# Softmax of the tap weights in three parts, two of them among the first products

## The reference, cut to what matters

```python
# x: (2, 3584, 192); weight_gen: (2, 3584, 8, 7)
w = weight_gen - np.max(weight_gen, axis=-1, keepdims=True)
w = np.exp(w)
w = w / (np.sum(w, axis=-1, keepdims=True) + 1e-09)
x_pad = np.concatenate([np.zeros((B, 6, D)), x], axis=1)
x_unf = x_pad[:, idx, :].reshape(B, S, 7, 8, 24)      # idx: seven rows up to this one
out = np.einsum('bshk,bskhg->bshg', w, x_unf).reshape(B * S, D)
# then: top 2 of 8 experts, relu(x @ w1[e]) @ w2[e], weighted;
# then: top 1 of 8 experts by cosine to their embeddings, the same products, weighted
```

## Time and profile before

| | |
|---|---|
| median of three runs | 1260.13 us |
| the three runs | 1262.2, 1260.13, 1260.13 us |
| the profiled execution | 1260.83 us |
| its span, first to last instruction | 1259.1 us |
| mean granted TensorE clock | 0.934 |
| busy over the span: TensorE, VectorE, ScalarE, GpSimd | 1095.6, 791.9, 553.8, 579.1 us |
| first product on VectorE | 20.33 us |
| last group's sum on VectorE | 119.86 us |

### The profile page before, as it was taken

The page is one execution under the profiler, slowest core; times in us unless marked ns, Lnnn a source line. Parts: engine busy times, 40 slices in busy tenths (PEclk is TensorE's granted clock), DMA queues, the critical chain, the costliest instruction groups (busy, mean ns, idle before and its releaser), DMA issues.

```text
span 1259.1 us, 27767 instructions
## 1 busy us (share of the span) xinstructions
PE 1095.6 (87%) x7950; PEld 1020.7 (81%) x7950; DVE 791.9 (63%) x1446; ACT 553.8 (44%) x1543; POOL 579.1 (46%) x676
## 2 busy tenths in 40 slices
PE   1899045899999999999999999968169999999997
PEld 1566012799999999999999999947049999999997
DVE  8998899545546464645545464466975655466763
ACT  2122155445445454544445354446554544455552
POOL 5778066344444444444444444400544444444444
PEclk9999555999999999999999999979569999999998
DMA  9111200311313131131313111164603313115421
GB/s 327 66 51 63 59 0 0 91 38 41 95 44 96 38 102 41 40 92 41 99 44 91 38 40 42 43 215 138 233 19 94 97 38 97 41 41 150 126 65 36
DMA packets 51185, 97.85 MB, mean 78 GB/s; under 512 B 9651, under 2 KB 33051, under 8 KB 50876
## 3 DMA queue, kind: packets, MB, share of 16 engines
q1 hardware_dynamic: 33084, 61.77, 16.3%
q0 software_dynamic: 18048, 35.42, 10.0%
HBM read 69.62 MB, written 29.10 MB: 78 GB/s over the span
## 4 chain that ended last, share of the span: by engine, by line
PE 76%; DVE 14%; issue 3%; POOL 2%; DMA 2%; ACT 1%; DVEq 1%; ACTq 0%; SPq 0%; POOLq 0%
PE banks L623 22%; PE banks L625 11%; PE banks L609 8%; PE banks L611 7%; PE banks L610 7%; PE banks L615 7%; PE banks L614 7%; DVE prods L874 3%; PE banks L534 2%; DVE lo_hot L974 2%; POOL prods L408 2%; PE banks L593 2%; PE banks L594 2%; DVE hi_eq L967 2%; PE banks L575 1%
## 5 line engine op out<-in xcount | busy, mean ns | idle before, releaser
L1042 DVE SCALAR_TENSOR_TENSOR h_lo<-banks,h_hi 128x256 fp32r<-128x256 f32 x736 | 312.5, 425 | 369.9 <-ACT h_hi L761 367.0
L761 ACT ACTIVATE h_hi<-banks 128x256 fp32r<-128x256 f32 x736 | 283.7, 385 | 451.3 <-PE banks L615 451.3
L623 PE MATMUL banks<-w_hl,h_hi 128*128 128x384 f32 x1472 | 468.3, 355 | 0.0
L625 PE MATMUL banks<-w_hl,h_lo 128*128 128x192 f32 x1472 | 370.7, 252 | 0.0
L625 PEld LDWEIGHTS banks<-w_hl,h_lo 128*128 128x128 f32 x1472 | 279.1, 190 | 0.0
L623 PEld LDWEIGHTS banks<-w_hl,h_hi 128*128 128x128 f32 x1472 | 276.6, 188 | 0.3
L433 POOL DMA_INDIRECT x_slots<-token_rows,gather_idx x192 | 194.2, 1012 | 105.3 <-POOL gather_idx L430 76.0
L609 PE MATMUL banks<-x_hi_a,w_hi 128*128 (+1 forms) x736 | 226.3, 308 | 1.8 <-DVE x_hl_b L1010 1.7
L610 PE MATMUL banks<-x_hi_a,w_lo 128*128 (+1 forms) x736 | 206.6, 281 | 0.0
L611 PE MATMUL banks<-x_lo_a,w_hi 128*128 (+1 forms) x736 | 206.1, 280 | 0.0
L614 PE MATMUL banks<-x_hl_b,w_hi 128*128 (+1 forms) x736 | 205.3, 279 | 0.0
(11 more groups left out here) (171 smaller groups left out, 1422.0 us busy)
## 6 DMA issues: line engine op xcount, KB each, us to landing
raw<-in_moe_w SPq DMA_DIRECT2D x17, 768.0 KB
choices<-choice_rows SPq DMA_DIRECT2D x28, 384.0 KB, 3.8
raw<-in_moe_w SPq DMA_DIRECT2D x17, 512.0 KB
raw<-in_moe_w SPq DMA_DIRECT2D x34, 256.0 KB
x_halo<-in_x SPq DMA_DIRECT2D x2, 2688.0 KB, 15.3
token_rows<-stage SPq DMA_DIRECT2D x14, 384.0 KB, 2.3
token_rows<-rows SPq DMA_DIRECT2D x14, 384.0 KB, 3.9
x_slots<-token_rows,gather_idx POOLq DMA_INDIRECT x192
```

The source lines that it names most:

```text
L623: mm(y[:, i, 0:2 * D], h_hi[:, c % HBUFS, t], w2_hl[u][:, c, :, :], start=c == 0, stop=False)
L625: ins = mm(y[:, i, 0:D], h_lo[:, c % HBUFS, t], w2_hl[u][:, c, 0, :], start=False, stop=c == FC - 1)
L761: sc.activation(h_hi[:, c % HBUFS, :], banks[:, c % HBANKS, 0:BLOCK], ACT.Relu).then_inc(h_hi_ready[m], 1)
L1042: v.scalar_tensor_tensor(h_lo[:, c % HBUFS, :], banks[:, c % HBANKS, 0:BLOCK], 0.0, h_hi[:, c % HBUFS, :].bitcast(F32), ALU.max, ALU.subtr ...
```

## The change

The softmax is cut into three parts, given by batch and tiles. Part 0 is tiles 0 to 7 of batch 0, the first two groups (448 elements per partition). Part 1 is the other 20 tiles of batch 0 (1120 elements). Part 2 is batch 1 (1568 elements). Part 0 is worked on VectorE and ScalarE ahead of the groups. For the other two GpSimd subtracts and scales, and VectorE takes maxima and sums among the groups' instructions: part 1 all in group 0; part 2's maximum in group 1 and its sum in group 3, scaled on GpSimd after group 4's additions. On ScalarE, part 1's exponential stands between the second and the third copy of weights, and part 2's ahead of `take_logits` and `take_turned` in the loop's first round (`g == 2`). The embeddings' square and root move into the round `g == 4`. Loads are issued in the order weights and rows of part 0, of part 1, of part 2, then the embeddings.

```diff
+    PARTS = ((0, 0, 2 * GROUP), (0, 2 * GROUP, J), (1, 0, J))
...
+        def part_first(g):
+
+            b, jj = divmod(g, GB)
+            return [i for i, (at, lo, _) in enumerate(PARTS) if (at, lo) == (b, jj * GROUP)]
+
+        def weight_part(i):
+
+            b, lo, hi = PARTS[i]
+            heads = slice(lo * H, hi * H)
+            return attn_w[:, b, heads, :], attn_red[:, b, heads], tap_sum[:, b, heads]
...
-            for b in range(B):
-                sp.dma_start(attn_w[:, b], weight_gen[b].rearrange("(p j) h k -> p (j h) k", p=P)).then_inc(attn_w_in[b], 16)
+            def load_weights(i):
+                b, lo, hi = PARTS[i]
+                rows = weight_gen[b].rearrange("(p j) h k -> p (j h) k", p=P)
+                sp.dma_start(weight_part(i)[0], rows[:, lo * H:hi * H, :]).then_inc(attn_w_in[i], 16)
+
+            def load_x(i):
+                b, lo, hi = PARTS[i]
+                if lo == 0:
+                    for first, end in ((1, 16), (16, P)):
+                        sp.dma_start(x_halo[first:end, b, 0:PAD], xt[b, first - 1:end - 1, J - PAD:, :]).then_inc(x_in[i], 16)
+                sp.dma_start(x_halo[:, b, PAD + lo:PAD + hi], xt[b, :, lo:hi, :]).then_inc(x_in[i], 16)
+
+            load_weights(0)
+            load_x(0)
+            load_weights(1)
+            load_x(1)
+            load_weights(2)
+            load_x(2)
             sp.dma_start(emb_sb[0:E], emb).then_inc(emb_in, 16)
-            for b in range(B):
-                sp.dma_start(x_halo[:, b, PAD:], xt[b]).then_inc(x_in[b], 16)
-                for lo, hi in ((1, 16), (16, P)):
-                    sp.dma_start(x_halo[lo:hi, b, 0:PAD], xt[b, lo - 1:hi - 1, J - PAD:, :]).then_inc(x_in[b], 16)
...
+            def center(i):
+                w, red, _ = weight_part(i)
+                pool.wait_ge(tap_max, i + 1)
+                gp.tensor_tensor(w, w, red.unsqueeze(2).to_broadcast(w.shape), ALU.subtract).then_inc(centered[i], 1)
+
+            def scale(i):
+                w, _, total = weight_part(i)
+                pool.wait_ge(exps, i + 1)
+                pool.wait_ge(tap_scale, i + 1)
+                gp.tensor_tensor(w, w, total.unsqueeze(2).to_broadcast(w.shape), ALU.mult).then_inc(weights_scaled[i], 1)
+
+            center(1)
             for g in range(NG):
...
+                if g == 0:
+                    scale(1)
+                if g == 1:
+                    center(2)
+                if g == 4:
+                    scale(2)
...
-            for b in range(B):
-                act.wait_ge(centered[b], 1)
-                sc.activation(attn_w[:, b], attn_w[:, b], ACT.Exp).then_inc(exps, 1)
-
-            act.wait_ge(emb_in, 16)
-            sc.activation(emb_sq[0:E], emb_sb[0:E], ACT.Square, accum_out=emb_norm[0:E, 0:1]).then_inc(act_step, 1)
-            act.wait_ge(act_step, 1)
-            sc.sqrt(emb_norm[0:E, 1:2], emb_norm[0:E, 0:1]).then_inc(emb_sumsq, 1)
-
+            def exp_weights(i):
+                w, _, _ = weight_part(i)
+                act.wait_ge(centered[i], 1)
+                sc.activation(w, w, ACT.Exp).then_inc(exps, 1)
+
+            exp_weights(0)
             take_weights(0)
             take_weights(1)
+            exp_weights(1)
             take_weights(2)
             take_turned(0, 0)
             for g in range(2, NG):
                 if g + 1 < NG:
                     take_weights(g + 1)
+                if g == 2:
+                    exp_weights(2)
                 take_logits(0, g - 2, 2 * E)
                 take_turned(0, g - 1)
+                if g == 4:
+                    act.wait_ge(emb_in, 16)
+                    sc.activation(emb_sq[0:E], emb_sb[0:E], ACT.Square, accum_out=emb_norm[0:E, 0:1]).then_inc(act_step, 1)
+                    act.wait_ge(act_step, 1)
+                    sc.sqrt(emb_norm[0:E, 1:2], emb_norm[0:E, 0:1]).then_inc(emb_sumsq, 1)
...
+            def taps_max(i):
+                w, red, _ = weight_part(i)
+                dve.wait_ge(attn_w_in[i], 16)
+                v.tensor_reduce(red, w, AX.X, ALU.max).then_inc(tap_max, 1)
+
+            def taps_sum(i):
+                w, _, total = weight_part(i)
+                dve.wait_ge(exps, i + 1)
+                step(v.tensor_reduce(total, w, AX.X, ALU.add))
+                step(v.tensor_scalar(total, total, 1e-9, None, ALU.add))
+                v.reciprocal(total, total).then_inc(tap_scale, 1)
+
+            w, red, total = weight_part(0)
+            taps_max(0)
+            dve.wait_ge(tap_max, 1)
+            v.tensor_tensor(w, w, red.unsqueeze(2).to_broadcast(w.shape), ALU.subtract).then_inc(centered[0], 1)
+            taps_sum(0)
+            dve.wait_ge(tap_scale, 1)
+            v.tensor_tensor(w, w, total.unsqueeze(2).to_broadcast(w.shape), ALU.mult).then_inc(weights_scaled[0], 1)
...
                 tap_products(g, 0, FIRST, first_prods)
+                if g == 0:
+                    taps_max(1)
                 tap_products(g, FIRST, SECOND, second_prods)
+                if g == 0:
+                    taps_sum(1)
+                if g == 1:
+                    taps_max(2)
+                if g == 3:
+                    taps_sum(2)
```

More of the change, by code:

```diff
@@ L178, in attention_moe_moe @@
         consts_ready = sem("consts_ready")
-        attn_w_in = [sem(f"attn_w_in{b}") for b in range(B)]
+        attn_w_in = [sem(f"attn_w_in{i}") for i in range(len(PARTS))]
         emb_in = sem("emb_in")
-        x_in = [sem(f"x_in{b}") for b in range(B)]
+        x_in = [sem(f"x_in{i}") for i in range(len(PARTS))]
         halo_zeroed = sem("halo_zeroed")
@@ L190, in attention_moe_moe @@
         emb_ready = sem("emb_ready")
-        centered = [sem(f"centered{b}") for b in range(B)]
+        centered = [sem(f"centered{i}") for i in range(len(PARTS))]
         tap_max = sem("tap_max")
         tap_scale = sem("tap_scale")
-        weights_scaled = [sem(f"weights_scaled{b}") for b in range(B)]
+        weights_scaled = [sem(f"weights_scaled{i}") for i in range(len(PARTS))]
         exps = sem("exps")
@@ L692, in take_weights @@
                 b, jj = divmod(g, GB)
-                if jj == 0:
-                    act.wait_ge(weights_scaled[b], 1)
+                for i in part_first(g):
+                    act.wait_ge(weights_scaled[i], 1)
                 if g >= 2:
@@ L848, in _ @@
                 v.memset(t[DB:P, :, 0:width], 0.0)
-            for b in range(B):
-                dve.wait_ge(attn_w_in[b], 16)
-                v.tensor_reduce(attn_red[:, b], attn_w[:, b], AX.X, ALU.max).then_inc(tap_max, 1)
-                if b == 0:
-                    dve.wait_ge(tap_max, 1)
-                    v.tensor_tensor(attn_w[:, b], attn_w[:, b], attn_red[:, b].unsqueeze(2).to_broadcast([P, J * H, K]),
-                                    ALU.subtract).then_inc(centered[b], 1)
-            for b in range(B):
-                dve.wait_ge(exps, b + 1)
-                step(v.tensor_reduce(tap_sum[:, b], attn_w[:, b], AX.X, ALU.add))
-                step(v.tensor_scalar(tap_sum[:, b], tap_sum[:, b], 1e-9, None, ALU.add))
-                v.reciprocal(tap_sum[:, b], tap_sum[:, b]).then_inc(tap_scale, 1)
-                if b == 0:
-                    dve.wait_ge(tap_scale, 1)
-                    v.tensor_tensor(attn_w[:, b], attn_w[:, b], tap_sum[:, b].unsqueeze(2).to_broadcast([P, J * H, K]),
-                                    ALU.mult).then_inc(weights_scaled[b], 1)
+            def taps_max(i):
[15 more added lines that the diff above has]
+            v.tensor_tensor(w, w, total.unsqueeze(2).to_broadcast(w.shape), ALU.mult).then_inc(weights_scaled[0], 1)
             dve.wait_ge(halo_zeroed, B)
@@ L886, in _ @@
             for g in range(NG):
-                if g % GB == 0:
-                    dve.wait_ge(x_in[g // GB], 48)
+                for i in part_first(g):
+                    dve.wait_ge(x_in[i], 48 if PARTS[i][1] == 0 else 16)
                 dve.wait_ge(w_in_psum, g + 1)
```

## The result

The changed kernel takes 1264.59 us (median of 8 runs, 1263.38 to 1266.11), the kernel before 1262.16 us (8 runs, 1260.13 to 1262.77): ratio 1.0024, 95% interval 1.0013 to 1.0034. It is 2.4 us slower, where 0.3 us faster was forecast. (The ratios with their intervals are the record's; they aren't the quotient of the two medians and differ from it by up to 0.08%, 1 us.) The profiled execution after took 1263.38 us (span 1261.7), the shortest of its eight; that of before, at 1260.83, was also near its lower end.

What follows compares the result with a forecast made beforehand. VectorE's full queue among the products was taken as the bound: 12 us of earlier start, minus 12.3 of softmax work and waits, plus a 0.56 wait gone, minus 0.3, gives 0.3 us faster, 1259.8 us; range 1257.4 to 1262.3.

Steps and rivals of the forecast that it cites:

- The rest at nothing: ScalarE's embeddings work in group 4, 2.3 us, hidden by 3.73 us waits for logits; load order also costs nothing.
- GpSimd's late additions in group 5: After GpSimd's scaling, group 5's additions start 1.5 us late; less 1.3 to spare, 0.3 us lost once.
- The start: First weights land at about 3.6, 4.4 us of softmax work follow, first product near 8.0 instead of 20.33.
- rival 3: Queued transfers share engines, so x's first piece is late; measurably slower from 10.8, 1265.5 at 13.7; chance 0.07.
- Part 1: Softmax work around group 0: VectorE waits 1.06 us for the exponential, loses 0.9 at the addition; group 1 begins at 19.65.
- the hold: VectorE's 1e-9 addition is held to the end of GpSimd's current instruction, losing 0.9 and 1.1 us.
- Part 2: Maximum after group 1, sum in group 3, 1.1 us lost at the addition; group 4 starts at 46.5, before 47.10.
- Rivals 1 and 2: First: no or hardly any holds, 1257.7, chance 0.15. Second: hold lasts over all additions in a row, 1261.6, chance 0.07.
- The exponential's place in ScalarE's queue: Third part's exponential is done at 34.0, needed at 40.7; behind the second copy of turned rows VectorE would wait 2 us.
- Rival 4: Earlier groups change something behind them, such as when TensorE's clock comes back; 3 us either way, chance 0.07.

Runs made afterwards that it cites:

- b_emb_late: The kernel before with only the embeddings' square and root moved behind the copy of turned rows in round 4: 1263.30 us against 1262.06, ratio 1.0012.
- weights_first: The changed kernel with ScalarE copying group g+2's weights between the logits and the turned rows: 1262.71 us against 1261.53 for the kernel before, ratio 1.0009.
- again: The changed kernel run once more without any edit: 1264.63 us against 1262.06 for the kernel before, ratio 1.0021.
- fill_only: The changed kernel with twelve filling products on TensorE ahead of its sums for groups 2 and 4: 1263.55 us against 1261.53 for the kernel before.
- fill: The changed kernel with the embeddings moved ahead of round 5's logits and twelve TensorE filling products for groups 2 and 4: 1263.74 us, ratio 1.0011 to before.
- x_merged: The changed kernel with the first piece of x and its halo read together in longer rows: 1266.74 us against 1262.06 for the kernel before.
- emb_early: The changed kernel with the embeddings' square and root moved ahead of ScalarE's wait for logits in round 5: 1263.61 us, ratio 1.0013 to the kernel before.

## Why the prediction was wrong

**The step that failed** is in "The rest at nothing": "its copy of weights is due a group later". I had read this from the code (one group's weights are copied in the round before) and had not looked at the clock times of the two rows at 45.43 and 46.13. The copy stands behind the copy of turned rows, which itself comes late in a group, and feeds a product 0.6 us after it ends. So ScalarE's 3.73 us waits for logits were no cover: the idle time lies in front of the chain logits, turned rows, weights, and the embeddings were put between its last two links. The square, load and root held the copy from 59.81 to 61.69; 1.9 us less 0.6 give the 1.28 us by which group 6 came late. b_emb_late shows it alone (1.2 us of time), weights_first shows it from the other side.

**The second loss was in no rival.** I followed VectorE's queue through its sum of the third part and asked what VectorE waits for, not who waits for VectorE. While it sums, GpSimd gets no products for 6.10 us (its idle time before 50.05) and TensorE has nothing for 4.5 us; the clock goes to half, and TensorE's group 4 comes late. That lateness too reaches VectorE mostly through the copy of weights: 1.6 us in the execution that shows it, nothing in the first profiled one, where the clock fell at another time, and between the medians of again and fill_only no more than their scatter.

**A term mis-sized.** GpSimd's late additions in group 5 were to cost 0.3 us. I had compared 1.5 us with the 1.3 to spare at the sum, where the tighter path, 0.6 at the weights, decides: 0.9 us in fill. In the changed kernel VectorE is so late already by then that this hides.

**Point by point.** The start: 3.8 us instead of 3.6 for the first weights, and 4.4 us of work from there, as worked out. (The rule of the Trainium skill, DMA: Bandwidth & Descriptors, Anatomy of one DMA, gave 3.3; the page states it for transfers that GpSimd issues, and these are SP's.) x came late, as rival 3 feared, though whether by its mechanism (the queued transfers share the engines) is not shown. It landed at 8.75, not at 6.9 to 7.9. Over the executions with the same loads the first product starts at 8.23 to 9.38, up to 0.9 us later than ScalarE's copy alone would allow. The place at which I said that it would decide, 10.8, was reached only in x_merged, which moved the loads (11.70, 4.7 us above its before). I had the halo's slow landing in the old rows (2.1 us for 571.5 KB) and gave it too little weight. Part 1: VectorE's wait for the exponential 0.97 us (1.06), the hold 0.8 beyond a free addition's 0.25 (0.9), from the first product to group 1's 11.55 (11.62). Part 2: from group 1 to group 4 26.73 (26.87), the hold to 1.38 (1.40). All this was right, and the Trainium skill's rule on the shared port (SBUF, Who interferes with whom) did its work for the forecast: both additions beside GpSimd were held, and one with GpSimd idle took 0.28. Rivals 1 and 2, no hold and a hold through all additions, are out. The exponential's place in ScalarE's queue mattered as said: 2.86 us of waiting instead of 2, of which 1.8 us net were lost. Rival 4, something behind the groups: the rest was 1.3 us longer in the first profile, from the last logits; whether the change has a part in that is open.

**The sum of the measured.** The first profile took 1263.38 us instead of the 1260.5 forecast for it: group 4 0.6 us later than forecast (x), 1.28 at the weights where 0.3 was forecast, 1.3 behind the groups, 2.9 in all. In the median execution (again) group 4 starts 0.5 us earlier than before (46.61 against 47.10), then 2.9 us are lost, 1.3 to the embeddings and 1.6 to the clock: 2.4 us slower at the last group's sum. The medians' 2.4 us consist of this and of what the rest behind the groups adds or spares in a typical execution, which the profiles don't settle. Shown alone is the embeddings' place, 1.2 us. Without the waits for weights (weights_first) the medians are 1.2 us apart, at the edge of what can be told from zero: that agrees with the small effect I had forecast, but doesn't confirm its 0.3, and the run has ScalarE's new order in it as well.

**What stays open:** why the first x came late, and whether transfers to partitions 16 to 127 take longer; whether the hold needs the fast mode; and how often the early and the late fall of the clock hit each kernel.

## What to carry to other kernels

For each instruction that is put into a queue, read from the timeline when the next one there ends and when its consumer starts, and take that difference as the cover: idle time elsewhere in the same queue is none. When a full engine gets a few us of other work in one piece, follow its consumers down to TensorE. And before adding work around a tight copy, ask whether the copy can stand earlier: here one reordering of ScalarE's queue took the waits that three different delays had made out of the profile.

## What the runs showed of the hardware

TensorE's granted clock fell to 0.50 in or just behind a stretch in which TensorE had nothing to do, at a moment that differs between executions of nearly the same work: at 33.6 (the first profile), 49.2 (again), 51.4 (emb_early), and at 52.6, 0.3 us after the work had resumed, in weights_first. A group's first eight matmuls then took 4.51 to 5.46 us instead of 3.23. In the gap of 3.21 us in front of group 4 in the first profile it did not fall. The Trainium skill (TensorE: Matmul & The Clock Gate, Part 1) says that the chip's watch runs freely of the kernel; the differing moments agree. While 1176 KB for 112 partitions were under way (x_merged), the transfers' engines were busy for 0.95 of the time at 240 GB/s from 3 to 9 us; at 10 to 11 us they moved 435. And VectorE's addition of 1e-9 took 0.28 us on 224 elements with GpSimd idle and 1.38 beside it, with a strided output 1.39.
